# Routing by batch inside attention, and two tiles of one expert ahead of the sort

## The reference

```python
# 1: attention, 8 heads of 64; heads 0-3 see a window of 32, heads 4-7 every 4th of 128
scores = where(mask, 0.125 * q @ k.T, -1e9); attn = softmax(scores); x = attn @ v
# 2: mixture of 8 experts, one expert for each token
logits = x @ w_gate                        # [b, s, 8]
local_gate = sigmoid(x @ w_local)          # [b, s]
for b, s:
    e = argmax(logits[b, s]) if s == 0 or local_gate[b, s] < 0.5 else prev_e
    prev_e = e
    out[b, s] = softmax(logits[b, s])[e] * (relu(x[b, s] @ w1[e]) @ w2[e])
# 3: gated causal convolution of 5 taps, then a projection
out = (sigmoid(conv5(x)) * (x @ w_val)) @ w_out
```

## Time and profile before

| | us |
|---|---|
| median of 3 runs | 599.38 (597.07 to 600.24) |
| the profiled execution, its own time | 598.12 |
| its span | 596.3 |
| TensorE busy | 546.2 (92%) |
| VectorE busy | 265.5 (45%) |
| ScalarE busy | 214.8 (36%) |
| GpSimd busy | 256.8 (43%) |

### The profile page before, as it was taken

How to read it: one execution, slowest core, us unless ns; L and a number is a source line. 1 busy time by engine, 2 the same in 40 slices (tenths; PEclk the granted TensorE clock), 3 DMA queues, 4 the chain that set the end, 5 groups by cost and what they waited for, 6 DMA issues and landing times.

```text
span 596.3 us, 10034 instructions
## 1 busy us (share of the span) xinstructions
PE 546.2 (92%) x3274; PEld 464.6 (78%) x3274; DVE 265.5 (45%) x833; ACT 214.8 (36%) x478; POOL 256.8 (43%) x161
## 2 busy tenths in 40 slices
PE   6899999972779999999999999999899487999997
PEld 3789989861658888788888888888687386999986
DVE  4577777754912121221212212122112689998710
ACT  2577777751012121121212112121112455565421
POOL 1000001381158555945276488684862425622210
PEclk8899999995889999999999999999999798999999
DMA  5758489869069996996998897989661512211112
GB/s 169 195 172 224 142 253 335 263 198 300 5 199 353 331 370 225 354 335 230 287 310 281 261 359 253 392 275 392 219 217 55 159 46 66 83 56 48 43 71 88
DMA packets 62772, 128.42 MB, mean 215 GB/s; under 512 B 9664, under 2 KB 17856, under 8 KB 62208
## 3 DMA queue, kind: packets, MB, share of 16 engines
q1 hardware_dynamic: 38560, 68.43, 35.5%
q0 software_dynamic: 17392, 46.93, 24.4%
q10 hardware_dynamic: 6768, 12.36, 6.1%
HBM read 104.28 MB, written 23.41 MB: 214 GB/s over the span
## 4 chain that ended last, share of the span: by engine, by line
PE 65%; DMA 15%; DVE 7%; POOL 6%; issue 4%; ACT 1%; SPq 1%; ACTq 0%; POOLq 0%; PEldq 0%; DVEq 0%
PE bank L1157 43%; PE bank L1174 7%; PE bank L1195 5%; DMA x_sorted<-gathered 4%; POOL w_low L564 3%; DMA stage<-in_moe_w 3%; DMA gathered<-x_tokens,token_idx 2%; PE bank L1183 2%; PE bank L1310 2%; DMA w_high<-in_moe_w 2%; PE bank L1218 2%; DMA kT<-in_k 2%; DVE gate_acc L970 2%; POOL gathered L600 1%; DMA vwin<-in_v 1%
## 5 line engine op out<-in xcount | busy, mean ns | idle before, releaser
L564 POOL TENSOR_TENSOR w_low<-stage,w_high 128x2048 fp32r<-128x2048 f32 x32 | 146.9, 4597 | 81.6 <-DMA stage<-in_moe_w 50.3
L1157 PE MATMUL bank<-w_high,x_high 128*128 x184 | 75.2, 409 | 6.4 <-POOL w_low L564 3.8
L1013 ACT ACTIVATE probs<-shifted,negmax 96x128 f32<-96x128 f32 x192 | 66.5, 394 | 39.7 <-PE bank L1183 24.1
L1157 PE MATMUL bank<-w_high,h_high 128*128 x184 | 73.7, 401 | 1.0 <-DVE h_low L931 1.0
L1157 PE MATMUL bank<-w_high,x_low 128*128 x184 | 73.0, 397 | 0.0
L1157 PE MATMUL bank<-w_low,x_high 128*128 x184 | 73.0, 396 | 0.0
L1157 PE MATMUL bank<-w_high,h_low 128*128 x184 | 72.0, 391 | 0.0
L1157 PE MATMUL bank<-w_low,h_high 128*128 x184 | 71.8, 390 | 0.0
L553 POOL DMA_DIRECT2D w_high<-in_moe_w x32 | 24.2, 768 | 103.2 <-DVE x_dil L739 85.5
L1054 ACT CAST x_high<-bank 128x512 fp32r<-128x512 f32 x25 | 14.7, 587 | 146.1 <-PE bank L1281 146.1
L917 DVE TENSOR_TENSOR x_low<-bank,x_high 128x512 fp32r<-128x512 f32 x25 | 17.3, 691 | 111.3 <-ACT x_high L1054 111.3
(11 more groups left out here) (184 smaller groups left out, 1056.7 us busy)
## 6 DMA issues: line engine op xcount, KB each, us to landing
w_high<-in_moe_w POOLq DMA_DIRECT2D x32, 1024.0 KB, 12.6
stage<-in_moe_w SPq DMA_DIRECT2D x32, 1024.0 KB, 7.6
y_sorted<-y_sb ACTq DMA_DIRECT2D x25, 256.0 KB, 6.9
vwin<-in_v SPq DMA_DIRECT2D x4, 1560.0 KB, 7.9
x_sorted<-gathered SPq DMA_DIRECT2D x21, 256.0 KB, 8.6
x_in<-x_sorted ACTq DMA_DIRECT2D x21, 256.0 KB, 5.9
kT<-in_k SPq DMA_DIRECT2D x32, 152.0 KB, 4.9
out<-o_sb SPq DMA_DIRECT2D x18, 256.0 KB, 2.0
```

Source lines behind the costliest of these rows:

```text
L564: g.tensor_tensor(low, stage[:, c % 2, :], high.bitcast(F32), ALU.subtract).then_inc(split_done, 1)
L1013: a.activation(probs[:, j % 2, u, :], shifted[:, j % 2, u, :], ACT.Exp, bias=negmax[:, j % 2, u:u + 1], scale=-1.0).then_inc(exp_done, 1)
L1157: ins = mm(dst, l, r, start=first and i == 0, stop=last and i == 2)
```

## The change

Batches 0 to 2 are routed while the next batch is in attention. The recurrence of batch b runs in five hops between VectorE and TensorE, one a step, beginning at `hop_step(b)`; GpSimd makes the best expert and the start rows (`fresh_choice`). A running count over the columns of the batches so far (`incl`) gives each token its rank within its expert at once, which does not depend on later batches. For expert 0 this rank is already the slot. Two tiles of it (`EARLY`) are taken early: tile 0 from batches 0 and 1, tile 1 from batches 0 to 2 (`EARLY_KNOWN`). Where expert 0 has fewer than 128 or 256 tokens by then, a column after the batch (`SEEN`) lifts its count, and the slots stay empty. To leave room the bodies go from 25 to 27.

TensorE does the first quarter of tile 0's up product ahead of the last gate products, and the other quarters and tile 1 between the hops of batch 3. ScalarE copies the two results unscaled (`early_y`); VectorE scales them later (`scale_y`). `keep_clock` during the routing is gone. Expert 0's weights are loaded and split during batches 1 and 2, expert 1's first raw chunks during batch 3, its high parts right after attention and ahead of the gathers. The fill of the unused rows of `y_sorted` moves from behind attention to the middle of batch 3. GpSimd makes its constants at the start, and makes the one-hot of a slot's low part (`low_one_hot`, 24 instructions) in place of VectorE. The first group of sorted gathers stays 5 tiles, the others become 3, 8 and 7 (before 5, 6 and 5). `qT` is split into two buffers and several small buffers move in SBUF.

```diff
--- before.py
+++ after.py
+EARLY = 2
+EARLY_KNOWN = (2, 3)
+ST = TOKENS // 128 + EXPERTS - 1 + EARLY
+SEEN = NQ + 1
+EARLY_STEP = STEPS * (BATCH - 1) + 5
...
+GATHERS = (range(DIRECT, 9), range(9, 12), range(12, 20), range(20, ST))
...
+        def hop_step(b):
+
+            return STEPS * (b + 1) + 7
+
...
+                if b == 0:
+                    load_raw(sp, 0, 0)
+                    load_raw(sp, 0, 1)
+                if b == 1:
+                    load_chunk(0, 2)
+                    load_chunk(0, 3)
                 if b == 2:
+                    for c in range(KD):
+                        rows = ys_dram[TOKENS:, c * 128:(c + 1) * 128].rearrange("(t p) c -> p t c", p=128)
+                        sp.dma_start(rows, ident[:].unsqueeze(1).broadcast_to([128, ST - TOKENS // 128, 128])
+                                     ).then_inc(y_filled, 16)
+                    load_chunk(1, 0)
+                    load_chunk(1, 1)
 
...
+            def fresh_choice(b):
+
+                t = of_batch(b)
+                po.wait_ge(top_ready, b + 1)
+                link(g.tensor_tensor(diff[:, t, :], logits[:, t, 0:EXPERTS], top[:, t].unsqueeze(2).broadcast_to(bte),
+                                     ALU.subtract))
+                link(g.tensor_scalar(cand[:], diff[:, t, :], 0.0, -float(EXPERTS), ALU.is_equal, ALU.mult))
+                g.tensor_tensor(cand2[:], cand[:], iota_e8[:].unsqueeze(1).broadcast_to(bte), ALU.add
+                                ).then_inc(cand_ready, 1)
+                link(g.tensor_scalar(gate1[:], logits[:, t, EXPERTS], KEEP_ABOVE, None, ALU.is_gt))
+                link(g.tensor_tensor(keep[:, t], gate1[:], not_first[:, t], ALU.mult))
+                link(g.tensor_scalar(anew[:], keep[:, t], -1.0, 1.0, ALU.mult, ALU.add))
+                po.wait_ge(fresh_ready, b + 1)
+                g.tensor_tensor(start[:, t], fresh[:], anew[:], ALU.mult).then_inc(rows_ready, 1)
+
+            def low_one_hot(first, last, batch_ranks):
+
+                po.wait_ge(ranks_ready, batch_ranks)
+                for t in range(first, last):
+                    ins = g.tensor_scalar(lo_hot[:, t, :], iota_lo[:], rank_parts[:, 0, t:t + 1], None, ALU.is_equal)
+                return ins
+
+            def early_members(tile):
+
+                n = NQ * EARLY_KNOWN[tile]
+                link(g.tensor_scalar(in_early[:, 0:n], rank_parts[:, 1, 0:n], float(tile), None, ALU.is_equal))
...
+                if tile:
+                    po.wait_ge(early_mm, tile)
+                link(g.tensor_tensor(early_tok[:, 0:n, 0], is_early[:, 0:n], iota_t[:, 0:n], ALU.mult))
+                g.tensor_scalar(early_tok[:, 0:n, 1], is_early[:, 0:n], iota_p[:], None, ALU.mult
+                                ).then_inc(early_ready, 1)
+
+            def early_gather(tile):
+
+                b = EARLY_KNOWN[tile]
+                po.wait_ge(plain_stored, 16 * b)
+                po.wait_ge(dil_stored, 16 * len(QUERY_PIECES) * b)
+                po.wait_ge(early_tokens, tile + 1)
+                gather(x_in[:, tile % 2, :], tile, x_dram[0:SEQ * b]).then_inc(xin_direct[tile % 2], 16)
+
...
+            po.wait_ge(normed, STEPS)
+            load_high(0, 0, 0)
+            fresh_choice(0)
+            split(0, 0, 0)
+            split(0, 1, 0)
+            po.wait_ge(normed, STEPS + STEPS // 2)
+            load_high(0, 0, 1)
+            fresh_choice(1)
+            split(0, 2, 0)
+            split(0, 3, 0)
+            po.wait_ge(scores_done, (BATCH - 1) * STEPS)
+            link(low_one_hot(0, 2 * NQ, 2))
+            early_members(0)
+            fresh_choice(2)
+            early_gather(0)
+            link(low_one_hot(2 * NQ, 3 * NQ, 3))
+            early_members(1)
+            early_gather(1)
+            po.wait_ge(pv_done, ALL_STEPS)
             po.wait_ge(dil_stored, 16 * len(QUERY_PIECES) * BATCH)
             load_high(1, 1, 0)
             load_high(1, 1, 1)
+            low_one_hot(3 * NQ, TT, 4).then_inc(lo_ready, 1)
+            po.wait_ge(plain_stored, 16 * BATCH)
+            po.wait_ge(token_ready, 1)
+
...
+            gather_direct(2)
+            gather_direct(3)
+            gather_sorted(0)
             gather_sorted(1)
             po.wait_ge(probs_ready, 1)
...
+            def rank_tokens(b):
+
+                dve.wait_ge(route_mm, 5 * b + 5)
+                at, col = hop_place(b, 4)
+                t = of_batch(b)
...
+                link(d.tensor_tensor(prod[:], got, ch[:, :, seen_in(b)], ALU.mult))
+                link(d.tensor_reduce(rank[:, t], prod[:].rearrange("p e t -> p t e"), AX.X, ALU.add))
+                link(d.tensor_copy(rank_i[:], rank[:, t]))
+                link(d.tensor_scalar(parts_i[:, 0, :], rank_i[:], 127, None, ALU.bitwise_and))
+                link(d.tensor_scalar(parts_i[:, 1, :], rank_i[:], 7, None, ALU.arith_shift_right))
+                d.tensor_copy(rank_parts[:, :, t], parts_i[:]).then_inc(ranks_ready, 1)
+                link(d.tensor_copy(batch_total[:, :, b], total))
+                if 1 <= b <= EARLY:
+                    link(d.tensor_scalar(lacking[:], total[0:1, 0:1], -1.0, 128.0 * b, ALU.mult, ALU.add))
+                    link(d.tensor_scalar(ch[0:1, 0, SEEN * b + NQ:SEEN * (b + 1)], lacking[:], 0.0, None, ALU.max))
+
+            def early_token(tile, at):
+
+                dve.wait_ge(early_mm, tile + 1)
...
+                for b in range(BATCH - 1):
+                    if s == hop_step(b) - 3:
+                        top_logit(b)
+                    if s == hop_step(b) - 2:
+                        first_of_best(b)
+                    if s == hop_step(b):
+                        scan_rows(b)
...
+                    if s == hop_step(b) + 4:
+                        rank_tokens(b)
+                if s == EARLY_STEP:
+                    early_token(0, 4 + EARLY_STEP % 2)
+                if s == ALL_STEPS + 2:
+                    low_x(0)
+
+
...
+            scan_rows(BATCH - 1)
+            carry_on(BATCH - 1)
+            early_token(1, 4)
+            choose_rows(BATCH - 1)
+            choose(BATCH - 1)
+            low_h(0)
+            low_x(1)
+            rank_tokens(BATCH - 1)
 
...
+                                 per_token(hi[:], ST), ALU.is_equal))
+            d.tensor_tensor(hi_tok[:, :, 0, :], hi_hot[:], per_token(iota_t[:], ST), ALU.mult)
+            d.tensor_scalar(hi_tok[:, :, 1, :], hi_hot[:], iota_p[:], None, ALU.mult).then_inc(hots_ready, 1)
+            low_h(1)
+            d.tensor_copy(expert_end[:], tend[:])
...
             act.wait_ge(y_filled, 16 * KD)
+            relu(0)
+            high_h(0)
             high_x(1)
+            relu(1)
+            early_y(0)
+            high_h(1)
+            early_y(1)
+            high_x(2)
+            high_x(3)
+            relu(2)
+            load_x(2, 0)
+            for s in range(EARLY + 1, ST + 1):
+                tile_step(s)
+                if s == EARLY + 1:
+                    for tile in range(EARLY):
+                        act.wait_ge(y_scaled, tile + 1)
+                        store_y(tile)
...
+            for s in range(ALL_STEPS + 5):
...
+                if s == ALL_STEPS:
+                    pe.wait_ge(shifted_done, UNITS * (ALL_STEPS - 1))
+                    transpose_x(0, 0)
+                if 4 <= s <= ALL_STEPS + 1:
+                    pe.wait_ge(normed, s - 3)
+                for b in range(BATCH - 1):
+                    if s == hop_step(b):
+                        transpose_rows_of(b)
...
+                    if s == hop_step(b) + 4:
+                        count_ranks(b)
+                if s == EARLY_STEP:
+                    find_early(0, 4 + EARLY_STEP % 2)
+                if s == ALL_STEPS + 2:
...
+                    early_up(0, 0)
+                if s >= 4 and s < ALL_STEPS + 4:
+                    gate_logits(s - 4)
+
+            last = BATCH - 1
+            early_up(0, 1)
+            pe.wait_ge(lg_taken, ALL_STEPS)
+            transpose_rows_of(last)
+            early_up(0, 2)
+            bring_ends(last)
+            find_early(1, 4)
+            early_up(0, 3)
+            bring_carry(last)
+            transpose_choice(last)
+            pe.wait_ge(early_tokens, EARLY)
+            transpose_hidden(0)
+            transpose_x(0, 1)
+            count_ranks(last)
+            for kk in range(KD):
+                early_up(1, kk)
+            early_down(0)
+            pe.wait_ge(hots_ready, 1)
+            pe.wait_ge(lo_ready, 1)
+            for t in range(TT):
+                ins = mm(bank[:, 7, 0:2 * ST], lo_hot[:, t, :], hi_tok[:, t, :, :].rearrange("p a s -> p (a s)"),
+                         start=t == 0, stop=t == TT - 1)
+            ins.then_inc(token_mm, 1)
+            transpose_hidden(1)
+            early_down(1)
+            pe.wait_ge(token_ready, 1)
+
...
             slot_probabilities()
-            transpose_hidden(0)
-            for s in range(1, TOKENS // 128):
```

(4 more changed lines are left out.)

630 lines of the change are left out of this document (351 added, 279 removed).

## The result

The changed kernel takes 624.17 us (median of 4 runs, 620.42 to 627.56) where the kernel before takes 599.11 (4 runs on the same chip): a ratio of 1.0425, 95% interval 1.0377 to 1.0473. It is slower by 4.25%, outside the range of 580 to 604 and on the other side of no change. The profiled execution took 620.42 us (span 618.7) against 598.12 (span 596.3), 22.4 us more in the span.

A forecast was written before the change was run, and what follows sets the result against it. TensorE was taken to bound attention (barely) and the expert stage, with a hole between. Attention +5.1, the hole -21.1, weights +4 and unused bodies +4.7 sum to -7.3 us: median 592 us, range 580 to 604.

The forecast's parts named there:

- Four splits beside batches 1 and 2 are charged nothing: Attention: GpSimd's splits, moved beside batches 1 and 2, add 0 us; doubled two-input VectorE instructions would add some 2 to 3.
- The kT wait: Attention, step 45: the 2.9 us wait for a kT load behind weight loads goes, counted as won.
- just fit: Attention, batches 1 and 2: 8 MB more over some 57 us (140 GB/s) fits beside 230 GB/s; a saturated stretch carries 349.
- Hops: Attention, batches 0 to 2: five hops each between TensorE and VectorE add 8 us in all; bounds 3 to 12.
- Attention to tile 3: From attention's end to up of tile 3: the hole closes, 24.1 us won, less 3 for slow clock: -21.1 us.
- some 42 were named as a sign: After attention: up of tile 2 starts some 42 us after the last attention product (36.8 plus hops and clock).
- The clock term: Attention to tile 3: slow clock behind idle gaps, 1.7 us a time, charged 3 us; bounds 1.7 and 8.
- Weights: Expert stage, experts 1 and 2: TensorE waits for late weights, 3 us at tile 6; +4 us charged, bounds 0 and 18.
- rival two: Tile 6: expert 2's raw chunks wait behind eight row stores, TensorE stands 18 us; 606 us, chance 0.12.
- Unused bodies: After the used tiles: two more unused bodies at 2.35 us each, set by hidden's cast and subtraction, +4.7 us.
- Rival four: Attention near step 41: a late split or one-hot makes TensorE wait, a miss by 8 us; 594 us, chance 0.1.
- Rival three: Routing and attention: slow clock through the routing and dear hops (8 and 12 us); 601 us, no change, chance 0.11.

The follow-up runs named there:

- the probes: Two kernels: the kernel before with one to three kinds of unused VectorE operations added in 15 attention steps; one run each, 606.83 and 605.23 us.
- after_again: The changed kernel run once more, with nothing changed; median 622.93 us.
- tiny_splits: The changed kernel with each of expert 0's four splits computing 16 of 2048 columns, its low parts mostly left zero; 2.7% above the kernel before.
- moved_weights: The kernel before with only expert 0's loads and splits moved under batches 1 and 2, routing as before; 1.15% slower than the kernel before.
- short_all: The changed kernel with expert 0's splits in pieces, numbers in PSUM, earlier one-hots, expert 2's raw chunks before row stores, 25 bodies; 1.015 of the kernel before.
- psum_hots: The changed kernel with rank digits' intermediate numbers in PSUM and one-hots made ahead of the second pair of splits; the time stayed, missing 607 to 611.
- raw_first: The changed kernel with expert 2's raw chunks 0 and 1 sent ahead of group 2's row stores; median not told from the changed kernel's.

## Why the prediction was wrong

**The step that failed** is "Four splits beside batches 1 and 2 are charged nothing". It rested on the normalising product, unchanged at 0.421 us beside the splits. But that product reads PSUM, and what the probes saw held are operations within SBUF. The change puts some ten of these per batch (four for the digits, four scans, the choice of rows, the lifted count) into the stretch where it also puts the splits. I had weighed a contention that doubles a duration, and only for operations with two SBUF inputs; what happens is that 0.17 us becomes the rest of a 4.5 us split, for a cast or a digit operation with one input too, and behind that wait the clock falls. Charged with nothing, the splits made TensorE wait 4.38 + 7.63 = 12.0 us in the profile after. Attention as a whole lost 10.5 us not busy and 6.9 of clock there (7.2 and 4.1 in after_again). Over the whole kernel the splits are worth some 9 us by tiny_splits, so this step is not all of the miss; the terms below are the others.

**The kT wait** of 2.9 us did go, but the bytes did not "just fit". The prediction's own numbers say so: 230 and 140 GB/s are 370, above the 349 that it took for a full stretch. And moved_weights waits for a store of x_dil, tiny_splits for lg_back, with a DMA share of 1.25 (90 to 100 us) and 1.18 (80 to 90 us) ahead of it. Of the 17.4 us of waiting and clock, moved_weights shows 8.0 without the hops, holds of its sum of logits among them. How the other 9.4 (3.3 in after_again) divide between lock and late one-hots varies from one execution to the next and stays open.

**Hops**: right in size, not in where they fall. TensorE's rest grew by 7.4 us, and by 8 to 10 in the other kernels with hops (8 in the forecast, and 2 or so for the first quarter tile and its transposes). I had laid most of it on VectorE and 0.6 us a batch on TensorE's own products. These products' durations, which overlap with others, add up to 6.5 us in the profile after, where 1.8 were charged.

**Attention to tile 3**: right in mechanism, 18.8 instead of 22.5 won. Up of tile 2 starts 39.3 us after the last gate product (196.48 and 157.16), where some 42 were named as a sign. The clock term was too small: the granted clock was 0.50 from 157.16 to 160 us, 0.77 to 165, and 0.66 in 185 to 190 and 195 to 200. Busy time times the missing clock makes 5.4 us of these four, where 3 were charged; no row had given the 1.7 us a time.

**Weights**: the wait is the one that the forecast and rival two both name, the raw chunk behind eight row stores. It was 8.0 us at tile 6 in the profiled execution, with 0.74 of clock in 240 to 260, and 3.8 to 5.7 for both places in others. The stretch cost 8.9 us instead of 4, far from rival two's 18. Raw chunks landed in a median of 8.8 us instead of the 7.6.

**Unused bodies**: the term of 4.7 us measured 8.5 to 9.7. I read the spacing of two bodies on ScalarE and took it as a rate. With four, TensorE's sequencer stands 2.4 to 3.3 us at single branches. Why a branch takes so long stays open.

Rival four named the place (a late split or one-hot within attention) and had 594, since it took the miss to be of GpSimd's time alone. Rival three had slow clock and dear hops, neither its cause nor its size. The sum with measured terms is 22.4 - 18.8 + 8.9 + 9.4 + 0.5 = +22.4 us.

## What to carry to other kernels

Before GpSimd work is moved under another stage, list the VectorE operations there that stay within SBUF, sums over groups left out: each can stand until a GpSimd instruction ends, 4.5 us here, so test the cost on one of these kinds. Check that the bytes moved under a stage fit by its own rates (370 against 349 GB/s here). In a stage with 0.1 us of margin a wait is paid twice, as idle time and as slow steps behind it, and mending one wait hands the time to the next in line. A count of empty loop bodies is priced by adding bodies, not from the spacing of two.

## What the hardware showed unexpectedly

Held operations differ in how they get their turn. Between back-to-back GpSimd instructions a cast or a digit operation gets in (0.65 us beside 0.69 us pieces). The sum of logits, a tensor_tensor with two SBUF inputs, doesn't: 9.93 us through 16 pieces (short_all), 7.35 through the boundary of two splits (psum_hots). Two inputs alone don't decide it: in raw_first the choice of rows, which reads two tensors from SBUF as well, stood from 107.41 to 111.87 us, with a boundary at 107.27 plus half of 8.99, 111.8. What does is open. Skipped tile bodies are not linear: the gap is 4.1 us with two, 12.6 with four.
